# Unit loads issued ahead of weights and operand stores, unit 10 in the early buffers, and product 1's split six slots later

## What is computed

```
kv  = einsum('bhsd,bhse->bhde', k, v)            # 8 x 8 heads, s = 576, d = 64
out = einsum('bhsd,bhde->bhse', q, kv)
x   = out / sqrt(mean(out*out, -1) + 1e-6) * g_norm    # -> x: 4608 tokens x 512
x   = (sigmoid(x @ w_gate) * (x @ w_val)) @ w_out      # 512 -> 1536 -> 512
x   = (silu(x @ w2_gate) * (x @ w2_val)) @ w2_out
```

## Time and profile before

| | us |
|---|---|
| median of 3 runs | 1835.38 (1835.14 to 1835.86) |
| profiled execution, device time | 1837.89 |
| its span in the trace | 1836.1 |
| PE busy in the span | 1758.0 (96%) |
| DVE, ACT, POOL busy | 1212.4, 897.3, 363.6 |
| first block's matmuls begin at | 70.80 |

### The profile page before, as it was taken

How to read it: one execution, slowest core, us unless ns; L and a number is a source line. 1 busy time by engine, 2 the same in 40 slices (tenths; PEclk the granted TensorE clock), 3 DMA queues, 4 the chain that set the end, 5 groups by cost and what they waited for, 6 DMA issues and landing times.

```text
span 1836.1 us, 30734 instructions
## 1 busy us (share of the span) xinstructions
PE 1758.0 (96%) x11184; PEld 1714.9 (93%) x11184; DVE 1212.4 (66%) x1897; ACT 897.3 (49%) x1687; POOL 363.6 (20%) x326
## 2 busy tenths in 40 slices
PE   6899999998999999999998999999999999999997
PEld 5788898998999999999998899998999999999997
DVE  3656756776756668765579777776766568655554
ACT  4555655554544445444445555555444445544444
POOL 5522222103311114211133100003211124111111
PEclk9999999999999999999999999999999999999999
DMA  7687587557656565656665455555655666455552
GB/s 181 193 244 224 166 280 237 179 196 232 221 195 209 189 213 198 226 194 206 205 211 204 182 192 193 195 191 203 236 190 189 204 227 225 150 185 190 187 183 71
DMA packets 199832, 366.93 MB, mean 200 GB/s; under 512 B 49665, under 2 KB 159745, under 8 KB 199681
## 3 DMA queue, kind: packets, MB, share of 16 engines
q1 hardware_dynamic: 199680, 364.96, 59.3%
HBM read 234.36 MB, written 130.55 MB: 199 GB/s over the span
## 4 chain that ended last, share of the span: by engine, by line
PE 76%; DMA 6%; DVE 5%; issue 5%; SPq 3%; POOL 2%; ACT 2%; DVEq 0%; POOLq 0%; ACTq 0%
PE ps L682 72%; DMA wops<-in_v_dram 2%; PE ps L586 1%; DMA wops<-in_moe_w_gate_dram 1%; PE ps L571 1%; DMA wops<-in_q_dram 1%; PE ps L624 1%; DVE arena L1131 1%; DVE hop L1088 1%; PE ps L576 1%; DVE xo L1015 1%; DVE wa L1010 1%; SPq L353 1%; POOL arena L1324 1%; DVE arena L1149 1%
## 5 line engine op out<-in xcount | busy, mean ns | idle before, releaser
L682 PE MATMUL ps<-xo,wa 128*128 128x384 f32 x6048 | 1090.1, 338 | 12.9 <-ACT arena L854 7.3
L682 PEld LDWEIGHTS ps<-xo,wa 128*128 128x128 f32 x6048 | 1052.8, 189 | 19.9 <-ACT arena L854 9.2
L1131 DVE TENSOR_TENSOR arena<-ps,arena 128x384 f32<-128x384 f32 x648 | 351.7, 553 | 375.0 <-PE ps L682 291.4
L854 ACT ACTIVATE arena<-ps 128x384 f32<-128x384 f32 x648 | 317.6, 491 | 575.8 <-PE ps L682 574.9
L682 PE MATMUL ps<-hop,wb 128*128 128x384 f32 x3024 | 547.0, 338 | 18.5 <-DVE arena L1149 8.4
L682 PEld LDWEIGHTS ps<-hop,wb 128*128 128x128 f32 x3024 | 527.4, 189 | 27.8 <-DVE arena L1131 8.3
L1088 DVE TENSOR_TENSOR hop<-arena,hop 128x384 fp32r<-128x384 f32 (+1 forms) x396 | 288.8, 752 | 47.7 <-ACT hop L836 42.0
L1324 POOL TENSOR_TENSOR arena<-arena 128x384 f32<-128x384 f32 x144 | 145.6, 1033 | 763.1 <-DVE arena L1131 762.9
L836 ACT ACTIVATE hop<-arena 128x384 fp32r<-128x384 f32 (+1 forms) x396 | 233.3, 609 | 73.1 <-DVE arena L1149 40.4
L868 ACT ACTIVATE arena<-arena 128x384 f32<-128x384 f32 x216 | 112.5, 521 | 67.6 <-DVE arena L1131 67.5
L1149 DVE TENSOR_TENSOR arena<-arena 128x384 f32<-128x384 f32 x216 | 129.9, 603 | 19.7 <-DVE arena L1131 0.5
(11 more groups left out here) (64 smaller groups left out, 830.6 us busy)
## 6 DMA issues: line engine op xcount, KB each, us to landing
xo<-x_operands SPq DMA_DIRECT2D x168, 768.0 KB, 6.4
x_operands<-xo SPq DMA_DIRECT2D x84, 768.0 KB, 4.8
x<-arena SPq DMA_DIRECT2D x120, 384.0 KB, 3.7
arena<-x SPq DMA_DIRECT2D x96, 384.0 KB, 4.3
xraw<-x SPq DMA_DIRECT2D x22, 768.0 KB, 6.3
out_dram<-wops SPq DMA_DIRECT2D x48, 192.0 KB, 2.1
wops<-in_k_dram SPq DMA_DIRECT2D x22, 288.0 KB, 5.1
wops<-in_v_dram SPq DMA_DIRECT2D x22, 288.0 KB, 5.5
```

Source lines behind the costliest of these rows:

```text
L682: mm = pe.matmul(dst, lhsT, rhs, start=(pr in (1, 5, 2) and c == 0 and i == 0), stop=(c == 1 and i == 2), skip_group_check=(pr in (6, 7, 4 ...
L854: nc.scalar.activation(dst, X(side), ACT.Copy).then_inc(copied, 1)
L1131: nc.vector.tensor_tensor(dst, acc, buf, ALU.add).then_inc(summed, 1)
```

## The change

Five edits. (1) `EARLY` is 11: unit 10 uses the buffers of the first units, and the two late buffers of the scaled output change places to fit; unit 11 is the first in `wops`. `late_unit` and `is_late` are rewritten so that they give what they gave. (2) SP's prologue issues units earlier and weights later; the six splits go to steps 4, 5, 6, 7, 9 and, for the sixth, into the first window on ACT, DVE and POOL. (3) In the loop SP issues `next_unit(u + 1)` ahead of `load_xraw` in window 0, and ahead of the stores of operands 5 and 6 in window 2. (4) In the first window the places of units 10 and 11 on PE and two copies on ACT move by one or two steps. (5) `split_x(nxt, 1)` in window 1 moves on ACT from slot 1 to slot 5 (ahead of the second weight split there), on DVE from before `total(11, 0)` to behind it.

```diff
-        EARLY = 10
+        EARLY = 11
-        o_late = [att_o[:], sg.rearrange("p i n -> p (i n)")[0:SP_]]
+        o_late = [sg.rearrange("p i n -> p (i n)")[0:SP_], att_o[:]]
-        W_STEP = {2 + i: i for i in range(6)}
+        W_STEP = {4: 0, 5: 1, 6: 2, 7: 3, 9: 4}
-        KVQ_0, O_0, XT_0 = {3: 9, 12: 10, 19: 11}, {7: 9, 15: 10, 22: 11}, {1: 7, 11: 8, 18: 9, 27: 10}
+        KVQ_0, O_0, XT_0 = {3: 9, 12: 10, 20: 11}, {7: 9, 16: 10, 24: 11}, {1: 7, 11: 8, 19: 9, 27: 10}
             load_unit(1)
+            load_unit(2)
             load_w(0)
-            load_unit(2)
+            load_unit(3)
             load_w(1)
-            for i in range(2, 6):
-                load_unit(i + 1)
-                load_w(i)
+            load_unit(4)
+            load_unit(5)
+            load_w(2)
+            load_unit(6)
+            load_w(3)
             load_unit(7)
             store_xT(4)
             load_unit(8)
+            load_w(4)
             store_xT(5)
+            load_unit(9)
+            load_w(5)
+            load_unit(10)
             store_xT(6)
-            load_unit(9)
-            load_unit(10)
             store_xo(0, 1)
+            store_xo(0, 2)
             store_xT(7)
-            store_xo(0, 2)
+            load_unit(11)
             store_xo(0, 5)
...
                 if is_late(u - 1) or qq == 0:
                     store_xT(u - 1)
+                next_unit(u + 1)
                 if prepares:
                     load_xraw(nxt, 0)
-                next_unit(u + 1)
...
+                next_unit(u + 1)
                 if prepares:
                     store_xo(nxt, X_ORDER[2])
-                next_unit(u + 1)
-                if prepares:
                     store_xo(nxt, X_ORDER[3])
...
                         unit_sq(9)
+                        split_w(5)
                         split_x(0, 7)
                         split_x(0, 4)
                         unit_xT(8)
                         split_x(0, 3)
                         copy(6, 0)
+                        unit_kv_qT(10)
                         copy(6, 1)
-                        unit_kv_qT(10)
...
                                 hop_split(2, 0)
-                                if prepares:
-                                    split_x(nxt, 1)
                                 if first_unit is not None:
...
                             if w == 1:
+                                if prepares:
+                                    split_x(nxt, 1)
                                 if first_unit is not None:
                                     split_w(first_unit + 1)
```

More of the change, by code:

```diff
@@ L312, in late_unit @@
         def late_unit(qq, w):
-            return EARLY + 2 * (WINDOWS * qq + w)
+            return SHARED + 2 + 2 * (WINDOWS * qq + w)
         def is_late(u):
-            return EARLY <= u < UNITS
+            return SHARED + 2 <= u < UNITS
         RES_AT = {11: (0, 0), 12: (0, 1), 21: (1, 0), 22: (1, 1)}
@@ L474, in next_unit @@
                 def next_unit(u):
-                    if is_late(u) and is_late(u + 1):
+                    if is_late(u) and EARLY < u + 1 < UNITS:
                         load_unit(u + 1)
@@ L903, in _ @@
                         unit_xT(9)
+                        copy(7, 1)
                         unit_kv_qT(11)
-                        copy(7, 1)
                         gated(22)
@@ L1207, in _ @@
                         total(11, 0)
+                        if w == 1 and prepares:
+                            split_x(nxt, 1)
                         total(22, 0)
@@ L1294, in _ @@
                     differences(W_STEP[t + 1])
-            for u in (8, 9):
-                rsqrt(u)
+            rsqrt(8)
+            differences(5)
+            rsqrt(9)
             for qq in range(QN):
```

## The result

The changed kernel took **1817.45 us** (median of 4 runs, 1817.03 to 1819.30), the kernel before, beside it, 1835.26 (4 runs, 1832.41 to 1835.86): ratio 0.9908, 95% interval 0.9891 to 0.9925, so 17.8 us less by the medians and 13.8 to 20.0 by the interval. The profiled execution has a span of 1815.4 us, against 1836.1: 20.7 less. 1812.1 was forecast, with 23.3 us of gain. Parts 1 and 3 came about as worked out, part 4 at half its size; what is missing is in part 2, block 0's first window.

The account below looks back on a forecast made before the run. TensorE, busy 96% of the span, bounds the kernel; only its waits and clock losses can be won. Gains 6.2, 0.2, 9.4, 6.3 and 1.2 sum to 23.3, off the 1835.4 median: 1812.1 us; 8-in-10 range 1806 to 1820.

Parts of the forecast that it names:

- Part 1: Prologue: units up to 5 issued before the first split wait; product 1 starts at 64.6, gain 6.2 us, bounds 3 to 9.1.
- Part 3: SyncE's order in the loop: six later waits for v go, 9.4 us, and with them the clock's drops, 6.3 us.
- part 4: Product 1's split six slots later: block 18 gains 0.8 us, block 17 0.4; together 1.2, bounds 0 and 3.
- part 2: Block 0's first window, with weight 4's and 5's splits added: gain 0.2 us, bounds minus 3 and plus 2.5.
- The 1.5 us at unit 8: Prologue: unit 8's load, behind the store of unit 4's xT, lands at 56.5 against 55.0 wanted, a 1.5 us wait.
- The rival that the prologue gives little: Prologue: the split-to-load loop remains and units 8 to 10 may slip; it gives 0 to 3, time 1817; chance 0.14.
- the clock going up in the prologue: Rival: denser prologue work raises the clock, steps after unit 6 shorten, some 5 us more go, 1807; chance 0.07.
- delays the block's first operand by 0.2: Block 0's first window: weight 4's split, beside xT and two steps of product 1, delays the first operand by 0.2 us.
- its 0.7 us: Block 0's first window: by the DMA page's fit unit 12 would be in time, giving about 0.7 us more.
- the bound of minus 3: Block 0's first window, lower bound: unit 12's 1.52 wait doubles and ScalarE's added split is not hidden.
- the rival on the other side: Slower: in blocks 0 to 3 `xraw` comes too late for product 1's split; 1844 at 8 us a block; chance 0.04.
- six waits made three drops: Loop's clock: six waits for v made only three clock drops, so the link is not one to one; bounds 0 and 7.

Follow-up runs that it names:

- the last two runs: Changed kernel with unit 12's load first, weight 4's low half later; plus weight 5's GpSimd differences over 2 columns: 1813.97 us; or product 1's old split in block 17: 1814.06.
- the half edits: Kernel before with only one window's part of the SyncE loop reordering: window 0 alone 1829.58 us (ratio 0.9962), window 2 alone 1829.06 us (0.9959).
- the last version above: Changed kernel with unit 12's load first, weight 4's low half later, product 1's split at its old place in block 17 alone, all operands computed: 1814.06 us.
- thin differences: Changed kernel with GpSimd's four differences for weight 5 over 2 of 256 columns, leaving three operands out: 1817.49 us, ratio 0.9902.

## Why the prediction was right or wrong, by its steps

**Part 1, the prologue: right.** Forecast: product 1 at 64.6, a wait of 4.8 at unit 6 (43.1). Measured: 64.16, and 4.09 at 42.51. The 1.5 us at unit 8 did not come from its load: steps 7 and 8 lost 0.56 and 1.13 waiting for VectorE's scaled outputs, at xT, and that this came to about the same was luck. The root before the second one took 4.00 us on GpSimd, beside a weight split of VectorE. The rival that the prologue gives little was wrong of product 1's start; of the clock going up in the prologue nothing is seen: PE ran from 19.50 to 38.42 without a gap, and each of the transposes at its end still took 1.22 us for six, which take 0.66 later at full clock (the granted clock has no record that early and prints 1.00).

**Part 2, the first window: this is the term that failed.** +0.2 was forecast and -2.6 came. Unit 12's waits shrank (0.23 + 0.71 left of 1.52), though its v, forecast for 102.4 (108.84 less 6.2 and 0.2), was waited for until 104.06. The mis-sized step is "delays the block's first operand by 0.2": I had weighed weight 4's and 5's splits on ScalarE and VectorE, and had left GpSimd's differences for weight 5 out of the count. Before, they were done ahead of product 1; now they lie beside VectorE's chain. The chain is 1.7 us longer for it, and 1.6 by the last two runs. The first operand came 0.7 later rather than 0.2, and the half clock added 0.7, which other traces of the old first window show as well. The fit of the Trainium skill that the prediction sets beside this part (page DMA: Bandwidth & Descriptors, section Anatomy of one DMA) is given there for transfers that GpSimd issues; this kernel's are issued by SyncE, so its 0.7 us had no ground here. The loss was inside the bound of minus 3, but that bound had been drawn from unit 12's wait and ScalarE, not from this.

**Part 3, the loop's order: right in sum.** 9.4 for the waits and 6.3 for the clock make 15.7; 16.3 measured. (Two small slips of the working change nothing: 142.84 to 148.22 is 5.4 us, not 5.3, and 786 kB at 236 GB/s take 3.3 us, not 3.2.) The waits from unit 16 on were 9.42 in all (1.92, 2.43, 1.93, 1.07, 1.85, 0.22), so the clock's share was 6.9. `xraw` came as forecast: ScalarE never waited for it in blocks 0 to 3, so the rival on the other side has no place in the trace. What I wrote of the link, that six waits made three drops and it is not one to one, the half edits bear out.

**Part 4: half the size, and block 18 not cleanly read.** 1.2 forecast, 0.6 measured: +0.94 in block 18 (0.8 forecast) and -0.37 in block 17 (+0.4 forecast, so with the wrong sign). In block 18 the copies did come 1.2 us sooner (1015.89 less 992.83, 995.11 less 973.27; 1.1 forecast), and PE then waited another 1.25 us at 999.78. But the kernel before also has a stretch of 3.4 us at half clock there (from 1016.4) and the changed one none. Without such a stretch the block takes 50.8 us with the split at its new place (six traces) and 51.5 at the old one (two), which would leave 0.7 for the split; two traces with the old place and the stretch take 51.0, so the size stays open. Block 17 is clearer: without half clock 52.2 at the old place (one trace), 52.8 to 53.1 at the new (six). ScalarE and GpSimd of the changed kernel there:

```profile
943.15 1.70 ACT L737 ACTIVATE wa<-wops 128x1792 fp32r<-128x1792 f32 x1 [2.35 <-POOL wops L1296]
```

```profile
940.71 2.41 POOL L1296 TENSOR_TENSOR wops<-wops 128x256 f32<-128x256 f32 x1
```

VectorE's weight split moved to 939.96, beside the last difference of the next weight, which took 2.41 where it takes 1.34 in the kernel before and 0.94 in the last version above; ScalarE's split of that weight waited for it, and PE waited 1.65 us for a copy at 945.28 where it had waited 0.52.

**Sum.** 6.6 - 2.6 + 16.3 + 0.6 = 20.9; with the 0.4 lost between 354 and block 17 and 0.2 gained behind block 18 it is the trace's 20.7. The timed runs say 17.8, with 13.8 to 20.0 by the interval; the 2.9 between them is that the profiled execution of before was 2.6 above its median and that of after 0.2 below its own. So of the 5.3 us between the forecast of 1812.1 and the measured 1817.45, 2.6 are the sum's (part 2 alone missed by 2.8), and the rest comes from taking a gain read in one trace, slower than the median, off the median.

## What to carry to other kernels

Ask of each moved piece of work what lies beside it on the other engines, not only what stands behind it in its own queue: here four preparing operations of GpSimd, moved from 53.68, ahead of product 1, to 72.94, stretched a chain of VectorE by 1.6 to 1.7 us. A wait is where the waiting engine meets a chain; moving the waiting instruction moves the wait, and only shortening the chain removes it. And undo parts in groups before trusting a sum: the prologue was worth nothing without the loop's order, and by the traces the two halves of the loop's order were worth 13 us one by one and 17 together.

## What the runs showed of the hardware that I had not expected

VectorE and GpSimd slow each other, both ways: fp32 operations of VectorE of 96x768 and 128x768 go from 0.95 us to 1.3 to 1.5 beside GpSimd's 128x256 subtractions, these from 0.72 to 1.3 to 1.45, and GpSimd's root on 96x12 took 4.84 us beside VectorE's weight split where it took 2.27 without. The Trainium skill, page SBUF — State Buffer, section SBUF: two separate sides, has a rule for it: an operation of VectorE with two inputs in SBUF and one of GpSimd that reads SBUF take a shared pair of ports in turn, and the other waits until the instruction ends. The traces agree in kind, since each slowed operation of VectorE is a tensor_tensor with both inputs there; the size they show is 0.3 to 0.5 us on each 0.95. They are not regular: beside the root VectorE's second operation took 1.36 us in the changed kernel and 0.96 with thin differences.

Stretches at half clock of 3.4, 6.8 and 10.2 us followed PE's waits at the block's start, and not in the order of the waits: 1.77, 3.36 and 4.56 us were followed by 3.4, 3.17 and 5.03 by 6.8, 4.28 by 10.2, and 1.59 in the kernel before by none. The differences between these variants in the first window are in part this, which is why a fix of 1 us there can't be judged from one run's time.
